# One step loop without drains, a per head product of k and v, and a reordered layer one, in a fused attention and two layer feed forward kernel

## The reference

```python
q_s = exp(q - max over d);  q_s /= sum over d + 1e-9
k_s = exp(k - max over s);  k_s /= sum over s + 1e-9
kv = einsum('bhsd,bhse->bhde', k_s, v)
x  = einsum('bhsd,bhde->bhse', q_s, kv)      # then [B * S, H * D] = [2304, 512]
h = x @ w_in1;  g = s * max(h, 0)**2 + b;  y = g @ w_out1
h = y @ w_in2;  g = h * tanh(log(1 + exp(h)));  out = g @ w_out2
```

## Time and profile before

| | |
|---|---|
| median of the runs | 889.38 us |
| profiled execution | 890.38 us, its span 888.6 us |
| PE (matmul) | busy 865.1 us, 97% |
| PEld (weight load) | busy 717.5 us, 81% |
| DVE | busy 613.5 us, 69% |
| ACT | busy 378.7 us, 43% |
| POOL | busy 26.6 us, 3% |
| granted TensorE clock, mean | 0.988 |

### The profile page before, as it was taken

One profiled execution on the slowest core, in us unless ns is written; L12 is line 12 of the kernel. 1 busy time (PEld: TensorE's weight loads), 2 busy tenths in 40 slices (PEclk: granted clock), 3 DMA queues, 4 the chain that ended last, 5 costly groups with the idle time before them and its releaser, 6 DMA issues.

```text
span 888.6 us, 11126 instructions
## 1 busy us (share of the span) xinstructions
PE 865.1 (97%) x4132; PEld 717.5 (81%) x4132; DVE 613.5 (69%) x1037; ACT 378.7 (43%) x621; POOL 26.6 (3%) x30
## 2 busy tenths in 40 slices
PE   9789999999999999999999899998999999999998
PEld 4578888888888888888997678897888788878886
DVE  8787776665475554222466889688797779778975
ACT  4445433332333323222356555455454445445443
POOL 2300000000000000000000000000000000000000
PEclk9799999999999999999999999999999999999999
DMA  9921111111111100000153000100000000000001
GB/s 227 339 53 40 25 29 28 41 41 41 41 40 40 40 0 1 1 1 0 49 190 143 1 0 1 48 1 1 25 1 0 12 36 0 0 28 19 0 0 48
DMA packets 60645, 36.15 MB, mean 41 GB/s; under 512 B 48320, under 2 KB 50368, under 8 KB 60608
## 3 DMA queue, kind: packets, MB, share of 16 engines
q1 hardware_dynamic: 60608, 35.66, 14.2%
HBM read 30.93 MB, written 4.72 MB: 40 GB/s over the span
## 4 chain that ended last, share of the span: by engine, by line
PE 80%; DVE 11%; ACT 6%; issue 2%; POOL 1%; DMA 0%; DVEq 0%; ACTq 0%
PE H L796 38%; PE Y L810 21%; PE Y L824 17%; PE H L763 2%; PE H L784 2%; ACT t L458 1%; DVE g L702 1%; DVE t L674 1%; ACT t L460 1%; DVE wout_lo L598 1%; DVE t L679 1%; ACT wout_hi L360 1%; DVE t L684 1%; PE H L775 1%; DVE win_lo L598 1%
## 5 line engine op out<-in xcount | busy, mean ns | idle before, releaser
L796 PE MATMUL H<-xs_hi,win_hi 128*128 128x512 f32 (+1 forms) x640 | 240.8, 376 | 7.7 <-DVE g_raw L697 3.3
L796 PE MATMUL H<-xs_hi,win_lo 128*128 128x512 f32 (+1 forms) x640 | 236.8, 370 | 0.0
L796 PE MATMUL H<-xs_lo,win_hi 128*128 128x512 f32 (+1 forms) x640 | 236.7, 370 | 0.0
L824 PE MATMUL Y<-wout_hi,g 128*128 128x512 f32 x576 | 190.1, 393 | 5.4 <-DVE g L702 5.4
L810 PE MATMUL Y<-g,wout_hi 128*128 128x512 f32 (+1 forms) x640 | 183.3, 371 | 0.7 <-DVE g L582 0.7
L796 PEld LDWEIGHTS H<-xs_hi,win_hi 128*128 128x128 f32 x640 | 121.4, 190 | 30.0 <-DVE g_raw L697 4.0
L796 PEld LDWEIGHTS H<-xs_hi,win_lo 128*128 128x128 f32 x640 | 121.3, 190 | 20.8
L796 PEld LDWEIGHTS H<-xs_lo,win_hi 128*128 128x128 f32 x640 | 121.4, 190 | 20.4
L824 PEld LDWEIGHTS Y<-wout_hi,g 128*128 128x128 f32 x576 | 108.7, 189 | 30.9 <-DVE g L702 8.7
L810 PEld LDWEIGHTS Y<-g,wout_hi 128*128 128x128 f32 x640 | 115.2, 189 | 20.1 <-DVE g L582 0.9
L577 DVE SCALAR_TENSOR_TENSOR g_raw<-g_raw,s_col 128x512 f32<-128x512 f32 (+1 forms) x80 | 55.5, 694 | 96.4 <-ACT g_raw L381 96.1
(11 more groups left out here) (73 smaller groups left out, 823.2 us busy)
## 6 DMA issues: line engine op xcount, KB each, us to landing
win_raw<-in_moe_w_in_dram SPq DMA_DIRECT2D x8, 1024.0 KB, 7.0
wout_raw<-in_moe_w_out_dram SPq DMA_DIRECT2D x8, 1024.0 KB, 7.3
g_flat<-in_v_dram SPq DMA_DIRECT2D x32, 144.0 KB, 3.3
out_dram<-xy SPq DMA_DIRECT2D x18, 256.0 KB, 2.1
qbuf<-in_q_dram SPq DMA_DIRECT2D x24, 144.0 KB, 2.8
kbuf<-in_k_dram SPq DMA_DIRECT2D x24, 144.0 KB, 2.9
raw<-in_k_dram SPq DMA_DIRECT2D x4, 288.0 KB, 3.9
raw<-in_q_dram SPq DMA_DIRECT2D x4, 288.0 KB, 6.1
```

What stands on the lines that cost most here:

```text
L796: last = nc.tensor.matmul(Hb[f % banks][:, 0:w], a[:, i, cols], m[:, i, 0:w], start=(i == 0 and n == 0), stop=(i == KC - 1 and n == XPASS ...
L824: last = nc.tensor.matmul(Y[i][:, :], g[:, f % LAG_B, a, rows], m[:, f, :], start=(f == 0 and n == 0), stop=(f == FC - 1 and n == XPASS - 1))
```

## The change

All steps of both layers are numbered by one counter c (0 to 159), and one loop in Python writes them out for each engine, without loops in the program. On PE the down product of step c - 3 or c - 4 follows the up product of step c across tile borders too, so no tile has a drain or a fill; only at the border of the layers three down products of layer one stand between the first up products of layer two. Layer one takes the tiles as 0, 1, 2, 4, 3. The input splits of the next tile move into the current tile's steps (`split_at`), hi has two buffers, and lo is written over the input in place. The copies of Y move to step 2 (layer one and first tile of layer two) or 3 of the next tile, and PE waits for them before the next tile's first down product. The units of attention start at the steps in START. The hi part of win 1 moves from before relu 0 to behind g_hi 0. `kv_product` multiplies each head for itself: 64 columns of k with 65 of v, into 64 partitions of the bank. The loads of SP are the same in the same order.

```diff
-        xy, _ = place("xy", [P, KC, N])
-        xs_hi, o = place("xs_hi", [P, KC, TILE], F32R)
-        xs_raw, _ = place("xs_raw", [P, KC, TILE], F32, o)
-        xs_lo, _ = place("xs_lo", [P, KC, TILE], F32R)
+        xy, o = place("xy", [P, KC, N])
+        xlo, _ = place("xlo", [P, KC, N], F32R, o)
+        xhi = []
+        for half in range(2):
+            here, o = place(f"xhi{half}", [P, KC, TILE], F32R)
+            xhi.append(here)
+            if half == 0:
+                xs_raw, _ = place("xs_raw", [P, KC, TILE], F32, o)
...
-        FIRST_HI = {2: ('out', 1), 4: ('in', 2), 6: ('out', 2), 8: ('in', 3), 10: ('out', 3)}
+        FIRST_HI = {0: ('in', 1), 2: ('out', 1), 4: ('in', 2), 6: ('out', 2), 8: ('in', 3), 10: ('out', 3)}
...
+        A_ORDER = (0, 1, 2, FULL, 3)
+        SRC = A_ORDER + B_ORDER
+        WIDTH = tuple(LAST if src == FULL else TILE for src in SRC)
+        BANKS = (KC,) * TILES + tuple(w // P for w in WIDTH[TILES:])
...
+        def slot(c):
+            return c % LAG_A if c < FC * TILES else (3, 2, 0, 1)[c % LAG_B]
+
+        def wait_used(engine, c):
+            if c % FC == FC - 1:
+                engine.wait_ge(y_ready, y_count(c // FC + 1))
+            else:
+                engine.wait_ge(g_used, (FC - 1) * (c // FC) + c % FC + 1)
+
+
+        START = {}
+        for batch in range(1, B):
+            for p in range(NP):
+                START[FC * (batch - 1) + (0, 4, 7, 10)[p] if batch == 1 else FC * (batch - 1) + (-3, 1, 5, 9)[p]] = (batch, p)
+
+        def unit_at(c):
+            return Unit(*START[c]) if c in START else None
+
+
+        def split_at(pos, f):
+            steps = (5, 9, 12, 15) if pos == 0 else (5, 8, 11, 14) if pos < TILES else (6, 8, 10, 12)
+            return steps.index(f) if pos + 1 < len(SRC) and f in steps else None
...
-            win_hi_part(0, 1)
...
+            for c in range(FC * TILES):
+                pos, f = c // FC, c % FC
+                if pos > 0 and f == LAG_A - 1:
+                    take_y(pos - 1)
+                relu(c, WIDTH[pos])
+                if unit_at(c - 1):
+                    q_exp(unit_at(c - 1))
+                if unit_at(c - 2):
+                    take_qT(unit_at(c - 2))
+                g_hi(c, WIDTH[pos])
+                if unit_at(c - 1):
+                    k_exp(unit_at(c - 1))
+                if pos == 0 and f in FIRST_HI:
+                    kind, i = FIRST_HI[f]
+                    hi_part(kind, 0, i)
+                if pos == FULL and f in NEXT_HI:
+                    kind, i = NEXT_HI[f]
+                    hi_part(kind, 1, i)
+                if split_at(pos, f) is not None:
+                    split_hi(pos + 1, split_at(pos, f))
...
+            for c in range(FIRST, END):
+                pos, f = c // FC, c % FC
+                rough_inverse(c, WIDTH[pos])
+                if pos == TILES and f == LAG_A - 1 or pos > TILES and f == LAG_B - 1:
+                    take_y(pos - 1)
+                if c + 1 < END:
+                    exp_h(c + 1, WIDTH[(c + 1) // FC])
+                if c > FIRST:
+                    g_hi_b(c - 1, WIDTH[(c - 1) // FC])
+                if pos == TILES and f in LATE_PARTS:
+                    kind, i = LATE_PARTS[f]
+                    hi_part(kind, 1, i)
+                if split_at(pos, f) is not None:
+                    split_hi(pos + 1, split_at(pos, f))
+            g_hi_b(END - 1, WIDTH[-1])
+            take_y(len(SRC) - 1)
...
-                for h in range(PAIR):
-                    rows = slice(h * D, (h + 1) * D)
-                    last = nc.vector.tensor_scalar_add(ksum[rows, n.p, :], bank[rows, (h + 1) * VW - 1:(h + 1) * VW], EPS)
+                last = nc.vector.tensor_scalar_add(ksum[:, n.p, :], bank[:, VW - 1:VW], EPS)
                 last.then_inc(ksum_done, 1)
                 dve.wait_ge(ksum_done, n.u + 1)
                 nc.vector.reciprocal(kinv[:, n.p, :], ksum[:, n.p, :]).then_inc(kinv_done, 1)
                 dve.wait_ge(kinv_done, n.u + 1)
                 for h in range(PAIR):
                     rows = slice(h * D, (h + 1) * D)
-                    last = nc.vector.tensor_scalar(kv[rows, n.p, h * D:(h + 1) * D], bank[rows, h * VW:h * VW + D],
+                    last = nc.vector.tensor_scalar(kv[rows, n.p, h * D:(h + 1) * D], bank[rows, 0:D],
...
+            for c in range(FC * TILES):
+                pos, f = c // FC, c % FC
+                w = WIDTH[pos]
+                if unit_at(c - 3):
+                    kv_norm(unit_at(c - 3))
+                if unit_at(c - 5):
+                    take_x(unit_at(c - 5))
+                if pos > 0 and f == LAG_A - 1:
+                    for i in (1, 3):
+                        take_y(pos - 1, i)
+                square(c, w)
+                if unit_at(c - 1):
+                    k_shift(unit_at(c - 1))
+                g_lo(c, w)
+                if unit_at(c - 1):
+                    q_sum(unit_at(c - 1))
+                    q_eps(unit_at(c - 1))
+                    q_inv(unit_at(c - 1))
+                    q_scale(unit_at(c - 1))
+                if unit_at(c):
+                    q_max(unit_at(c))
+                    q_shift(unit_at(c))
+                    k_max(unit_at(c))
+                if pos == 0 and f in FIRST_LO:
+                    kind, part = FIRST_LO[f]
+                    lo_part(kind, 0, part)
+                if pos == FULL and f in NEXT_LO:
+                    kind, part = NEXT_LO[f]
+                    lo_part(kind, 1, part)
+                if split_at(pos, f) is not None:
+                    split_lo(pos + 1, split_at(pos, f))
...
+            def ratio(c, w):
+                dve.wait_ge(a_done, c - FC * TILES + 1)
+                if c >= FC * TILES + LAG_B:
+                    wait_used(dve, c - LAG_B)
+                elif c > FC * TILES:
+                    wait_used(dve, c - LAG_A - 1)
...
+            for c in range(FIRST, END + 2):
+                pos, f = c // FC, c % FC
+                w0, w1, w2 = [WIDTH[min(c - back, END - 1) // FC] for back in range(3)]
+                if FIRST < c <= END:
+                    rough_ratio(c - 1, w1)
+                if c < END:
+                    min_e(c, w0)
+                if FIRST < c <= END:
+                    unity(c - 1, w1)
+                leave = pos - 1 if c < END and f == (LAG_A if pos == TILES else LAG_B) - 1 else None
+                if c >= FIRST + 2:
+                    g_lo_b(c - 2, w2)
+                if leave is not None:
+                    take_y(leave, 1)
+                if c < END:
+                    m_of_e(c, w0)
+                if leave is not None and BANKS[leave] == KC:
+                    take_y(leave, 3)
+                if FIRST < c <= END:
+                    ratio(c - 1, w1)
+                    gate(c - 1, w1)
+                if pos == TILES and f in LATE_PARTS:
+                    kind, i = LATE_PARTS[f]
+                    lo_part(kind, 1, i)
+                if c < END and split_at(pos, f) is not None:
+                    split_lo(pos + 1, split_at(pos, f))
+            for i in (1, 3):
+                take_y(len(SRC) - 1, i)
...
-                    last = nc.tensor.matmul(n.bank[0][:, 0:PAIR * VW], n.kj[:, j, :], n.v[:, :, j, :],
-                                            start=(j == 0), stop=(j == J - 1))
+                    for h in range(PAIR):
+                        rows = slice(h * D, (h + 1) * D)
+                        last = nc.tensor.matmul(n.bank[0][rows, 0:VW], n.kj[:, j, rows], n.v[:, h, j, :],
+                                                start=(j == 0), stop=(j == J - 1))
...
+                if f == 0 and pos > 0:
+                    pe.wait_ge(y_taken_act, y_count(pos) // 2)
+                    pe.wait_ge(y_taken_dve, y_count(pos) // 2)
...
+            FIRST, END = FC * TILES, FC * len(SRC)
+            for c in range(FIRST):
+                if unit_at(c - 5):
+                    x_product(unit_at(c - 5))
+                n = unit_at(c - 3)
+                if n and n.u > NP:
+                    q_transpose(n)
+                if c >= HA:
+                    pe.wait_ge(ha_taken, c - HA + 1)
+                up(c, HA)
+                if n and n.u == NP:
+                    q_transpose(n)
+                elif n:
+                    kv_product(n)
+                if c >= LAG_A:
+                    down_a(c - LAG_A)
+                if n and n.u == NP:
+                    kv_product(n)
+
+            for c in range(FIRST, END + LAG_B):
+                if c < END:
+                    if c < FIRST + HB:
+                        pe.wait_ge(ha_taken, min(c - HA + 1, FIRST))
+                    else:
+                        pe.wait_ge(hb_taken, c - FIRST - HB + 1)
+                    up(c, HB)
+                if c < FIRST + LAG_A:
+                    down_a(c - LAG_A)
+                if c >= FIRST + LAG_B:
+                    down_b(c - LAG_B)
```

(66 more changed lines are left out.)

324 lines of the change are left out of this document (102 added, 222 removed).

## The result

The changed kernel takes 901.87 us (median of 4 runs, 900.13 to 902.62), where the kernel before took 890.74 beside it: ratio 1.012, interval 1.0088 to 1.0151. It is 1.2% slower; the forecast was 883.6 us and faster. The profiled execution has a span of 900.8 us, 12.2 more.

The account below looks back on a forecast made before the run. It took TensorE as the bound, busy 865.1 of 888.6 us. 888.6 - 16.8 + 7.8 + 0.5 + 1.5 + 1.2 = 882.8 us span, plus 1.8 around it, less 1.0 for the runs' median: 883.6. Range 876 to 892.

Parts of the forecast that it names:

- Part 4: Layer one's attention units started closer together: DVE stays under PE, so cost 0 (up to 3) us.
- the cover: Layer one, units three steps apart: 16.3 us of steps hide the 11 to 15 us chain from unit start to q_scale.
- Rival C: Stalls come back elsewhere, including transposes of units at 7, 10, 13, 0.7 late each: 5.6 more, 889.2 us; chance 0.23.
- Part 1: Drains removed, narrow tile fourth, wide last: 16.8 us of stalls and half clock gone, 7.8 put back, 0.5 new half clock.
- It just fits: Layer two's narrow tile: DVE has 4.3 us spare for 4.1 of added splits and copies, so 0 stall.
- 1.6 behind it: Layer two, border from narrow to wide tile: first down product waits for the copy on ACT, stall 1.6 us.
- Part 2: Start of layer one, reordered: stall moved to the first transposes, 0.7 us later, with half clock +1.5 (-0.3 to +3.3).
- the half clock behind it: Start, after 4.3 us idle before the first transposes: about four matmuls at double pitch, 0.8 us.
- Part 3: k and v product per head: +0.1 us a unit, twelve units on PE's path in layer one, +1.2 (-8.0 to +14.4).
- My line: Head product: pass time follows its columns, 0.84 to 0.87 ns each, so 24 passes take 1.34 us as before.
- rival A: Head product: both heads run side by side, each unit 0.67 us cheaper, 9.2 less, 874.4 us; chance 0.15.
- the upper bound: Head product: 24 passes at 0.083 us plus an emptied array twice, at most 0.27 each: +1.2 us a unit.

Follow-up runs that it names:

- Experiment 4: The changed kernel with the attention units' work on DVE and ACT in the order of the kernel before: 893.82 us against 890.95 for the kernel before.
- experiment 6: Experiment 4 plus win 1's hi part back before relu 0, units every four steps, x product and take_x earlier, last chunk split inside step 15: 888.93 us.
- Experiment 7: The changed kernel with DVE's lo split of the next tile in layer two one step later: 895.28 us against 890.95 for the kernel before.
- experiment 2: The changed kernel with the k and v product of both heads together again: 904.47 us against 890.95 for the kernel before.
- experiment 8: Experiment 7 plus, in layer two, ACT's copies of Y ahead of the step's Ln and Exp: 889.54 us against 892.68 for the kernel before.
- experiment 1: The kernel before with only the k and v product per head, heads alternating: 887.88 us against 890.95 for the kernel before.
- experiment 3: As experiment 1, but all six passes of one head ahead of the other's six: 894.18 us against 891.24 for the kernel before.
- experiment 9: The changed kernel with the changes of experiment 6 and experiment 8 together: 877.38 us against 892.68 for the kernel before.

## Why the prediction was wrong

**Part 4 failed, and decided the sign.** I took 0 (up to 3) for the closer units; they and their new order cost some 14.5 us (11.8 in steps 8 to 19, 2.7 in the later units, the borders of the head product aside). The step that fell is the cover: 3 steps of 16.3 us against a chain of 11 to 15 from a unit's start to its q_scale. In the trace of after:

```profile
87.02 2.95 PE Y L786 x12
...
90.06 0.61 ACT g_raw L404
...
94.75 1.49 DVE kmax L509
96.24 2.20 DVE wout_lo L595
...
102.14 0.95 DVE qbuf L523
...
103.12 0.83 DVE xy L560 x2
...
104.09 0.69 PE H L746 x6
```

The chain itself is 13 us (90.06 to 103.09), in the band. But it starts late: relu of a step waits for the down product three steps back (`g_used`), which ends at 89.98, a whole product (2.7 us) behind the up product from which I counted. That is as before; what is new is that square and g_lo now stand ahead of the unit's maxima, and that the sum comes a step later. And the transposes wait for take_x of the unit before as well (`x_taken`), which stands behind all of it on DVE. I had named the transposes' wait for q_scale only. Experiment 4 shows that order carries a part, and experiment 6 that with the distance undone too (and the x product earlier) the waits go. Then came what I had allowed nothing for here: half clock, twice, behind 2.2 and 2.8 us of idle time.

Rival C had this place, at 0.7 us a unit, where the three units cost about 4 each.

**Part 1: half failed.** Over the end of layer one and layer two the excess went from 16.9 to 13.7, so 3.2 gained where I had 8.5. Right: no drain is left, the steps 4 to 11 of layer two have 1.5 and 1.9 where I had 1.9 and 2.1, wide to wide is 0.8 and 0.8, as forecast. Wrong: the 0 for the narrow tile ("It just fits"), which has 3.6, 0.6 of it forecast for the copies at its start; and 1.6 behind it, which became 5.1 with half clock. I had summed DVE's busy time: 25.3 of every 28 us leave 4.3 in the tile, for 4.1 of new work. Busy time was not the limit: the split makes DVE wait for ACT (26.7 us in all, 15 times, both layers together, in the waits of after), and with its instructions in a fixed order DVE does nothing else meanwhile. Experiment 7 takes 6.3 us of it away by one step's delay of the same instructions.

**Part 2: the stall right, half clock mis-sized.** PE stands idle 4.03 us before 57.99, where I had 4.3. The first up product is at 41.16 here and at 40.13 before, so the transposes come 16.8 us behind it, where they came 16.3 behind it before (56.41): 0.5 later, and I had 0.7. The term that was wrong is the half clock behind it. I had counted 0.8, four matmuls at double pitch; in this trace the granted clock is 0.51 from 57 to 64 us, and the excess of the start grew by 3.5, not 1.5. The first down product shows it: 5.06 us for 12 matmuls that take 2.72 at full clock.

```profile
57.99 1.22 PE H L746 x6
59.21 5.06 PE Y L786 x12
```

Some of this is the execution that was profiled. In the traces of experiments 2 and 8, with the same code there, the clock is back after half that time and the start's excess is 7.6 and 7.8: 2.2 to 2.4 more than before, nearer to my 1.5.

**Part 3: mis-sized, some 4.5 us in favour.** I had +1.2; the runs show -3.1 (experiment 1), -2.6 (experiment 2 against after) and, by the steps' length, -3.4. My line (columns set the time) holds for the passes of one head, 0.057 us each (experiment 3). In alternating order the two heads overlap, as rival A had it: two passes start 4 to 8 ns apart, a pair every 56 to 61 ns. The borders, which I had put into the upper bound with 0.27 each for an emptied array, cost 0.1 each; that it is the emptying that takes this time is not shown. The Trainium skill, TensorEngine Tiling (Array Packing), section Tiling Modes, has both rules, the independent tiles and the drain at a change of mode; the runs show the first and are in keeping with the second. The overlap saves 0.49 us a unit, the borders take back 0.21.

**The sum.** -16.8 + 7.8 + 0.5 should have been -3.2 (5.3 worse), the start +3.5 (2.0 worse), the product -3.3 (4.5 better), the units +14.5 (14.5 worse), and the first matmul's 1.0: 12.5 us more instead of 5.8 less. The last item is chance as far as the runs tell, and so is about 1 of the start's 3.5.

## What to carry to other kernels

Before moving work of a lagging engine, walk one instance of it through every semaphore its consumer waits for, and start the walk where the producer's own wait ends, not where its input is ready; busy shares hide both. Where two engines hand a piece to each other inside one step, let the second take it a step later: the same instructions, 6 us less here. A stall of 2 or 3 us can have half clock behind it, here 1.5 to 3 us more: price both, as a chance and not as a certainty, and read a single trace with that in mind.

## What the runs showed of the hardware

Two float32 products of 64 weight columns into different 64 partitions, issued in turns, ran side by side: 24 passes of 65 columns in 0.85 us, against 1.36 in the order of one head after the other, and 1.34 for 12 passes of 130 columns and all 128 weight columns. Going into and out of this mode cost 0.1 us each way between full size matmuls.

The granted clock fell behind idle times of TensorE of 2.2, 2.8, 3.3 and 4.0 us in the trace of after and of 2.88 us before, and not behind one of 1.25. But the length of the idle time alone doesn't decide it. In the trace of experiment 6 the clock stayed at 1.00 behind 3.33 us (shown there); in that of experiment 9 it fell behind 1.58 us:

```profile
63.09 0.70 PE L761 MATMUL H<-xy,kv 128*128 128x288 f32 x1 [1.58 <-DVE kv L556]
...
63.00:67.40 4.40, 4.32 (x11) 3.26 (x12) 2.97 (x4) 1.36 (x3) 0.00 (x0) 0.61 0.59 132
```

Behind like stalls of 4.0 us it was 0.51 over the next 7 us in after and 0.75 in experiment 8.
